# The low-part score products of the alone pairs on 64 rows of the array

## The chip, the cores and the metric

The kernel runs on one core of one Trainium2 chip. The metric is the device time of one execution in microseconds; the time of a kernel is the median of its runs.

## What is computed

Attention with capped scores over 4 x 12 heads, 448 positions and head width 64, followed by two gated products over all 1792 tokens. The reference, cut to what matters:

```python
scores = scale * np.matmul(q, k.transpose(0, 1, 3, 2))
scores = cap * np.tanh(scores / cap)
scores = scores - np.max(scores, axis=-1, keepdims=True)
attn = np.exp(scores)
attn = attn / (np.sum(attn, axis=-1, keepdims=True) + 1e-09)
x = np.matmul(attn, v)                      # heads put side by side: 1792 x 768

gate = 1.0 / (1.0 + np.exp(-(x @ w_gate)))  # 768 x 1536
x = (gate * (x @ w_val)) @ w_out            # 1536 x 768
h = x @ w_in                                # 768 x 2048
y = (h * np.cos(h)) @ w_out2                # 2048 x 768
```

All of it is float32.

## The kernel before

**Two parts for one number.** A float32 operand is split into a high part, rounded to the type fp32r, and a low part, the rest. A product of the gated stages is then three products on TensorE (`block3`: high x high, high x low, low x high).

**The scores** need only two, since the contraction is over 64 numbers and the array has 128 rows. `qk` brings q and k of a head twice, in partitions 0 to 63 and in 64 to 127. In place, q becomes (high part in partitions 0 to 63, low part in 64 to 127). This is done by one subtraction, L391: the tile `q_hi` is zero in partitions 0 to 63 and holds the high part of q in 64 to 127, and `q - q_hi` rounded to fp32r is just that. k becomes `k_hh` (the high part in both halves) and, in place, k's low part in both halves. A product with `k_hh` (L506) gives (q high + q low) x k high, a product with k's low part (L507) gives (q high + q low) x k low. Both contract over all 128 rows.

**Pairs, tiles, groups.** Two heads make a pair (`pr`, with d = 0, 1 for the head). The 896 queries of a pair are 7 tiles of 128; tile 3 (`MID`) takes the last 64 queries of either head, so it has products of both heads. The tiles go in groups (`GROUPS`): part 0 is tiles 0 and 1, part 1 tiles 2 and 3, part 2 tiles 4 and 5, part 3 tile 6. The scores of a group go into two PSUM banks, one for each tile (n = 0, 1), 448 columns each. Counted in products, a pair has 4 + 6 + 4 + 2 = 16.

**The alone pairs.** The six pairs of batch 0 (`pr < ALONE`) are worked on ahead of everything else, in steps of a software pipeline (`alone(m)`, one on each engine). In step m TensorE does the transposes of the first tile of group m-3, the scores of group m+1 (into `s_ps` or the first two banks of `acc`, in turn), products with v of an earlier pair (`times_v_alone`, plain float32, L561), and the transposes of the second tile. ScalarE takes tanh, then exp of every tile; VectorE takes the row maximum (L1091), the reciprocal of the sum, the normalisation (L1119) and a part of the copies of transposed tiles (L970), GpSimd the other normalisations and the splits of q and k. The later batches' pairs are worked on beside the gated products of the batch ahead; they call the same `scores`.

**Order and waits.** Each engine's order is as written, and semaphores tie the engines together. `scores` waits for the splits of the pair (`s_qk`, `s_first_low`), the caller for the tanh that frees the banks (`s_tanh`). GpSimd starts with the identity matrix for the transposes, then splits the second head of pair 0 and the first of pair 1. VectorE zeroes `q_hi` and splits the very first head. There is one `q_hi` for all pairs; GpSimd and VectorE alone use it. `z_hi` is a tile for the output of the second gated product, 128 partitions by 6 x 448 numbers, and is first written long after the alone pairs.

Of the kernel before, what the change touches and what calls it, by code (L numbers as in the profile page):

```python
# [11 lines left out]
ALU = mybir.AluOpType  # L12
# [3 lines left out]
B, H, S, D = 4, 12, 448, 64  # L16
DM = H * D
FF1, FF2 = 1536, 2048
P = 128
# [6 lines left out]
GROUPS = ((0, 1), (2, 3), (4, 5), (6,))  # L26
NG = len(GROUPS)
MID = 3
LAST = S // P * P
GAP = P - S % P  # L30

TURN = S - LAST
KW = TURN + S
# [7 lines left out]
ALONE = PAIRS  # L41
# [23 lines left out]
def build(nc, qk, v0, v, w1, w2, w3, w4, yT):  # L65

    def sb(name, shape, dtype=F32):
        return nc.alloc_sbuf_tensor(name, shape, dtype)
# [10 lines left out]
    def sem(name):  # L79
        return nc.alloc_semaphore(name)  # L80

    def f32(tile):
        return tile.bitcast(F32)
# [4 lines left out]
    z_hi, z_lo = sb("z_hi", [P, KD, S], F32R), sb("z_lo", [P, KD, S], F32R)  # L88
# [10 lines left out]
    k_hh = [[sb(f"k_hh{p}{d}", [P, KW], F32R) for d in range(2)] for p in range(2)]  # L99
    q_hi = sb("q_hi", [P, S + GAP], F32R)  # L100
# [8 lines left out]
    rowsum, guarded, recip = sb("rowsum", [P, TILES, 2]), sb("guarded", [P, TILES]), sb("recip", [P, TILES])  # L109

    prob_alone = [h_lo_whole[:, TILES * p:TILES * (p + 1), :] for p in range(2)]
    pt_alone = [h_hi_whole[:, 8 * p:8 * (p + 1), :].rearrange("p (c e) s -> p c (e s)", e=2) for p in range(2)]
# [17 lines left out]
    zeros = [bank[:, 511:512] for bank in o_ps]  # L132

    s_const, s_capd, s_zero, s_ident = sem("consts"), sem("cap_derived"), sem("ident_zeroed"), sem("ident_ready")
    s_pad = sem("zeros")
    s_wld = [[sem(f"w_whole_loaded{p}{h}") for h in range(2)] for p in range(LO)]
    s_whi, s_wsplit = sem("w_hi_done"), sem("w_split")
    s_hikept = [[sem(f"w_hi_kept{p}{h}") for h in range(2)] for p in range(HI)]
# [4 lines left out]
    s_khi, s_qhi, s_qk = [sem(f"k_hi_done{d}") for d in range(2)], [sem(f"q_hi_done{d}") for d in range(2)], [sem(f"qk_split{d}") for d in range(2)]  # L143
    s_first_kld, s_first_k = sem("k_of_first_head_loaded"), sem("k_hi_of_first_head")
    s_first_qhi, s_first_low = sem("q_hi_of_first_head"), sem("low_parts_of_first_heads")
    s_v0ld, s_vld = [sem(f"v_alone_loaded{d}") for d in range(2)], [sem(f"v_loaded{d}") for d in range(2)]
    s_vhi, s_v = [sem(f"v_hi_done{d}") for d in range(2)], [sem(f"v_split{d}") for d in range(2)]
    s_score, s_tanh, s_max, s_shift = sem("scores_done"), sem("tanh_done"), sem("max_done"), sem("shift_done")
# [17 lines left out]
    def keys(pr, d, of=qk_in):  # L166
        return of[pr % 2][d][:, K_AT[d]:K_AT[d] + KW]

    def queries(pr, d, of=qk_in):

        return of[pr % 2][d][:, KW:KW + S] if d == 0 else of[pr % 2][d][:, 0:S + GAP]

    def turned(pr, t):

        return t > MID if pr < ALONE else t in [ts[1] for ts in GROUPS if len(ts) > 1]

    def keys_of(pr, t):

        return slice(0, S) if turned(pr, t) else slice(TURN, KW)

    def tile_queries(pr, t, d):

        at = KW + P * t if d == 0 else LAST if t == MID else P * (t - MID - 1)
        return qk_in[pr % 2][d][:, at:at + P]

    def columns(pt, chunks, t):

        if t == MID:
            return pt[:, chunks, :].rearrange("p c (d s) -> p c d s", d=2)[:, :, :, LAST:S]
        at = P * t if t < MID else S + P * (t - MID - 1)  # L190
        return pt[:, chunks, at:at + P]
# [74 lines left out]
    with block:  # L266
# [114 lines left out]
        def _(e):  # L381
# [2 lines left out]
            e.affine_select(out=ident[:, :], in_=ident[:, :], compare_op=ALU.not_equal, fill=1.0,  # L384
                            base=0, pattern=[[-1, P]], channel_multiplier=1).then_inc(s_ident, 1)

            def rounded(out, in_):
                return e.tensor_scalar(out, in_, 1.0, 1.0, ALU.mult, ALU.mult)  # L388

            def rest(out, whole, hi):  # L390
                return e.tensor_tensor(out, whole, f32(hi), ALU.subtract)  # L391

            def qk_high(pr, d):

                q = queries(pr, d, qk_whole)
                e.wait_ge(s_qkld[pr % 2][d], 16 * (pr // 2 + 1))
                if pr == 0:
                    e.wait_ge(s_ident, 1)
                    e.wait_ge(s_first_low, 1)
                else:  # L400
                    rounded(k_hh[pr % 2][d][:, :], keys(pr, d, qk_whole)).then_inc(s_khi[d], 1)
                    e.wait_ge(s_khi[d], pr)
                rounded(q_hi[D:P, 0:q.shape[1]], q[D:P, :]).then_inc(s_qhi[d], 1)
                e.wait_ge(s_qhi[d], pr + d)

            def qk_low(pr, d):
                q = queries(pr, d, qk_whole)
                if pr > 0:
                    rest(keys(pr, d), keys(pr, d, qk_whole), k_hh[pr % 2][d][:, :])
                rest(queries(pr, d), q, q_hi[:, 0:q.shape[1]]).then_inc(s_qk[d], 1)  # L410

            def split_qk(pr, d):
                qk_high(pr, d)
                qk_low(pr, d)
# [9 lines left out]
            def split_v(pr, d):  # L424
                e.wait_ge(s_vld[d], 16 * (pr - ALONE + 1))
                if pr > ALONE:
                    e.wait_ge(s_pv, 2 * (pr - 1) + d + 1)
                rounded(v_hl[d][:, :, 0, :], v_raw[d][:, :, :]).then_inc(s_vhi[d], 1)
                e.wait_ge(s_vhi[d], pr - ALONE + 1)
                rest(v_hl[d][:, :, 1, :], v_raw[d][:, :, :], v_hl[d][:, :, 0, :]).then_inc(s_v[d], 1)  # L430
# [40 lines left out]
            for m in range(STEPS + 1):  # L471
                if m > 0:
                    normalise(m - 1)
                pr, d = divmod(m // 2 + 3, 2)
# [17 lines left out]
        def _(e):  # L492

            def scores(g, to):
                pr, part = divmod(g, NG)
                if part < 2:
                    if pr > 0 or part > 0:
                        e.wait_ge(s_qk[part], pr + part)
                    if pr == 0:
                        e.wait_ge(s_first_low, part + 1)  # L500
                for n, t in enumerate(GROUPS[part]):
                    heads = [d for d in range(2) if (t <= MID, t >= MID)[d]]
                    for d in heads:
                        q, last = tile_queries(pr, t, d), d == heads[-1]
                        k_hi, k_lo = k_hh[pr % 2][d], keys(pr, d)
                        e.matmul(to[:, n, 0:S], q, k_hi[:, keys_of(pr, t)], start=(d == heads[0]), stop=False)  # L506
                        m = e.matmul(to[:, n, 0:S], q, k_lo[:, keys_of(pr, t)], start=False, stop=last)  # L507
                m.then_inc(s_score, 1)

            def bank_is_free(x):  # L510
# [401 lines left out]
        @block.vector  # L912
        def _(e):
            e.memset(half_pi[:, :], math.pi / 2).then_inc(s_const, 1)
            e.memset(f32(q_hi)[0:D, :], 0.0).then_inc(s_pad, 1)
            for zero in zeros:
                e.memset(zero, 0.0).then_inc(s_pad, 1)
            e.memset(f32(qk_in[1][0])[:, KW + S:QK], 0.0).then_inc(s_pad, 1)
# [7 lines left out]
            first_keys(0)  # L926
            q = queries(0, 0, qk_whole)
            e.wait_ge(s_qkld[0][0], 16)
            e.tensor_scalar(q_hi[D:P, 0:S], q[D:P, :], 1.0, 1.0, ALU.mult, ALU.mult).then_inc(s_first_qhi, 1)
            e.wait_ge(s_first_qhi, 1)  # L930
            e.tensor_tensor(queries(0, 0), q, f32(q_hi)[:, 0:S], ALU.subtract).then_inc(s_first_low, 1)
            e.wait_ge(s_capd, 1)
            e.tensor_scalar(rowmax[:, :, 1], cap_abs[:, :].to_broadcast([P, TILES]), -1.0, None, ALU.mult).then_inc(s_const, 1)
            e.reciprocal(cap_inv[:, :], cap_abs[:, :]).then_inc(s_const, 1)
# [260 lines left out]
```

## Time and profile before

| | us |
|---|---|
| median of 3 runs | 1247.42 |
| lowest, highest | 1245.74, 1247.77 |
| the profiled execution | 1248.63 |
| its span, first to last instruction | 1246.8 |
| TensorE busy | 1233.1 |
| VectorE busy | 640.2 |
| ScalarE busy | 517.6 |
| GpSimd busy | 410.7 |
| end of the alone pairs | about 84 |

How to read the views: the page gives busy times over the whole span, the view by stretch the same for parts of it. The chain of waits follows the work that ended last back in time, and lists what it went through. The timeline lists single instructions. In it "PE" is a TensorE product and "PEld" the load of its weights, 128*128 the part of the array, and the shape behind it the output. A product's duration reaches from its start to the modelled end of its last column, so the products of a row overlap; the distance of two starts is what one costs. DVE is VectorE, ACT ScalarE, POOL GpSimd. The granted clock of TensorE is 1.00 in every stretch shown.

### The profile page before, as it was taken

How to read it: one execution, taken by the hardware profiler on the slowest of the kernel's cores; microseconds unless marked ns; L12 is line 12 of the kernel's file. 1: busy time of each engine (PE TensorE's matmuls, PEld its weight loads, DVE VectorE, ACT ScalarE, POOL GpSimd, SP SyncE). 2: the span in 40 equal slices, each digit the busy share in tenths (PEclk: the TensorE clock that was granted, in tenths of full speed). 3: DMA queues.
4: the chain of work that ended last, by engine and by line, in shares of the span. 5: the costliest groups of instructions: out<-in, count | busy, mean ns of one | idle time of the engine just before them, and what ended most of it. 6: DMA issues, size and time to landing. Idle time of an engine off the chain costs nothing.

```text
span 1246.8 us, 17228 instructions
## 1 busy us (share of the span) xinstructions
PE 1233.1 (99%) x6246; PEld 1120.9 (90%) x6246; DVE 640.2 (51%) x1332; ACT 517.6 (42%) x1051; POOL 410.7 (33%) x410
## 2 busy tenths in 40 slices
PE   7999999999999999999999999999999999999999
PEld 5779989999899999999999999999999999999998
DVE  6951158866772226876675212787666411114610
ACT  7941155555641116555652112665664111104510
POOL 7969968799653102322002300334100000000000
PEclk9999999999999999999999999999999999999999
DMA  4478986799677665456645665556654466666663
GB/s 153 159 239 317 321 299 233 257 329 327 231 277 277 212 222 193 168 204 233 249 159 197 234 224 205 176 192 229 223 218 173 143 233 213 218 215 216 243 234 113
DMA packets 100452, 279.19 MB, mean 224 GB/s; under 512 B 11152, under 2 KB 19600, under 8 KB 100368
## 3 DMA queue, kind: packets, MB, share of 16 engines
q1 hardware_dynamic: 96912, 272.58, 62.5%
q10 hardware_dynamic: 3456, 5.51, 1.2%
q8 instruction: 51, 0.84, 0.3%
q14 instruction: 33, 0.27, 0.1%
HBM read 219.05 MB, written 58.98 MB: 223 GB/s over the span
## 4 chain that ended last, share of the span: by engine, by line
PE 93%; DVE 3%; ACT 2%; issue 1%; DMA 0%; POOL 0%; SPq 0%; ACTq 0%
PE acc L592 26%; PE acc L591 26%; PE acc L593 26%; PE t_ps L543 3%; PE s_ps L506 2%; PE acc L581 2%; PE s_ps L507 2%; PE acc L561 2%; PE acc L583 2%; PE t_ps L527 1%; DMA qk_in_whole<-qk 0%; DVE rowmax L944 0%; ACT prob L752 0%; PE t_ps L545 0%; ACT h_lo_whole L773 0%
## 5 line engine op out<-in xcount | busy, mean ns | idle before, releaser
L591 PE MATMUL acc<-h_hi,w_hi 128*128 128x448 f32 x672 | 251.1, 374 | 0.0
L592 PE MATMUL acc<-h_lo,w_hi 128*128 128x448 f32 x672 | 245.8, 366 | 0.0
L593 PE MATMUL acc<-h_hi,w_lo 128*128 128x448 f32 x672 | 245.3, 365 | 0.0
L591 PE MATMUL acc<-x_hi,w_hi 128*128 128x448 f32 x576 | 211.3, 367 | 0.0
L593 PE MATMUL acc<-x_hi,w_lo 128*128 128x448 f32 x576 | 210.7, 366 | 0.0
L592 PE MATMUL acc<-x_lo,w_hi 128*128 128x448 f32 x576 | 210.7, 366 | 0.0
L1028 DVE SCALAR_TENSOR_TENSOR acc<-scratch,acc 128x448 f32<-128x448 f32 x48 | 30.2, 629 | 232.1 <-PE acc L593 232.0
L591 PE MATMUL acc<-z_hi,w_hi 128*128 128x448 f32 x384 | 140.7, 366 | 0.1
L593 PE MATMUL acc<-z_hi,w_lo 128*128 128x448 f32 x384 | 140.5, 366 | 0.0
L592 PE MATMUL acc<-z_lo,w_hi 128*128 128x448 f32 x384 | 140.5, 366 | 0.0
L593 PEld LDWEIGHTS acc<-h_hi,w_lo 128*128 128x128 f32 x672 | 126.3, 188 | 10.0
L591 PEld LDWEIGHTS acc<-h_hi,w_hi 128*128 128x128 f32 x672 | 126.4, 188 | 9.3
L592 PEld LDWEIGHTS acc<-h_lo,w_hi 128*128 128x128 f32 x672 | 126.5, 188 | 8.9
L391 POOL TENSOR_TENSOR w_lo<-w_lo_whole,w_hi 128x768 fp32r<-128x768 f32 (+1 forms) x64 | 125.1, 1954 | 5.3
L592 PEld LDWEIGHTS acc<-x_lo,w_hi 128*128 128x128 f32 x576 | 108.2, 188 | 9.2 <-issue 0.2
L593 PEld LDWEIGHTS acc<-x_hi,w_lo 128*128 128x128 f32 x576 | 108.2, 188 | 9.1
L591 PEld LDWEIGHTS acc<-x_hi,w_hi 128*128 128x128 f32 x576 | 108.2, 188 | 9.0 <-issue 0.2
L388 POOL TENSOR_SCALAR k_hh<-qk_in_whole 128x512 fp32r<-128x512 f32 x46 | 29.1, 633 | 241.0 <-DMA qk_in_whole<-qk 241.0
L830 ACT ACTIVATE h_hi<-acc 128x448 fp32r<-128x448 f32 x48 | 26.2, 545 | 178.6 <-DVE acc L1028 178.6
L758 ACT ACTIVATE prob<-prob,shift,cap_abs 128x448 f32<-128x448 f32 x126 | 94.6, 753 | 11.9 <-DVE shift L946 11.9
L944 DVE TENSOR_REDUCE rowmax<-prob 128x2 f32<-128x896 f32 x72 | 69.7, 968 | 55.7 <-ACT prob L752 55.6
L796 ACT ACTIVATE pt_hi<-t_ps 128x512 fp32r<-128x512 f32 (+1 forms) x126 | 68.3, 542 | 63.9 <-PE t_ps L543 38.4
(110 smaller groups left out, 2025.0 us busy)
## 6 DMA issues: line engine op xcount, KB each, us to landing
w_lo<-w_pair SPq DMA_DIRECT2D x156, 384.0 KB, 3.8
w_hi<-w_pair SPq DMA_DIRECT2D x156, 384.0 KB, 3.0
w_lo_whole<-w SPq DMA_DIRECT2D x52, 384.0 KB, 3.8
w_pair<-w_lo SPq DMA_DIRECT2D x52, 384.0 KB, 4.3
w_pair<-w_hi SPq DMA_DIRECT2D x52, 384.0 KB, 4.8
w_lo<-w_pair SPq DMA_DIRECT2D x36, 512.0 KB, 4.4
w_hi<-w_pair SPq DMA_DIRECT2D x36, 512.0 KB, 3.3
qk_in_whole<-qk SPq DMA_DIRECT2D x24, 512.0 KB, 5.7
```

Of the source, the lines that this page charges most:

```text
L388: return e.tensor_scalar(out, in_, 1.0, 1.0, ALU.mult, ALU.mult)
L391: return e.tensor_tensor(out, whole, f32(hi), ALU.subtract)
L506: e.matmul(to[:, n, 0:S], q, k_hi[:, keys_of(pr, t)], start=(d == heads[0]), stop=False)
L543: m = e.transpose(t_ps[x % 2][:, bass.ts(c, P)], p[:, first + c * P:first + (c + 1) * P], ident[:, :])
L591: e.matmul(out[:, 0:S], w_hi[u % HI][:, wb, :], a_hi[:, kb, :], start=first, stop=False)
L592: e.matmul(out[:, 0:S], w_hi[u % HI][:, wb, :], a_lo[:, kb, :], start=False, stop=False)
L593: return e.matmul(out[:, 0:S], w_lo[u % LO][:, wb, :], a_hi[:, kb, :], start=False, stop=last)
L758: e.activation(prob[:, t, :], prob[:, t, :], ACT.Exp, bias=shift[:, t:t + 1], scale=cap_abs[:, 0:1], accum_out=rowsum[:, t, 0:1]).then_inc ...
L796: e.activation(columns(pt_hi, slice(0, n), t), chunks_of(t_ps[x % 2], n, t), ACT.Copy).then_inc(s_pthi, 1)
L830: e.activation(h_hi[:, j, :], acc[2 + p][:, 0:S], ACT.Copy, scale=0.5).then_inc(s_hhi, 1)
L944: e.tensor_reduce(rowmax[:, at, 0], prob[:, at, :], AXIS_X, ALU.max).then_inc(s_max, 1)
L1028: e.scalar_tensor_tensor(acc[2 + p][:, 0:S], tmp_a[p], 1.0, acc[2 + p][:, 0:S], ALU.add, ALU.mult).then_inc(s_gated, 1)
```

## The change

In the alone pairs, in groups of two tiles, `scores` hands over to a new function `scores_alone`. It issues the products with the high part of k first, for all tiles of the group. Then it issues those with the low part, but over 64 rows only. Tile 0 of the group takes partitions 0 to 63: there q's high part lies in place. Tile 1 takes partitions 64 to 127, and there the high part of q comes from the rounded copy that `q_hi` held. (The product q low x k low falls away.) That copy must now last until TensorE has read it, so four areas of `z_hi` (`q_hi_alone`, two pairs by two heads) take the place of `q_hi` for the alone pairs. Their partitions 0 to 63 are zeroed once, in three of them and in `q_hi` by GpSimd, in one by VectorE, which formerly zeroed `q_hi`; two gaps of 64 columns in partitions 64 to 127 are zeroed too. The groups of one tile, and all pairs of later batches, stay as they were. The diff, without the signal's declaration:

```diff
+    q_hi_alone = [[z_hi.rearrange("p k s -> p (k s)")[:, (S + GAP) * (2 * p + d):(S + GAP) * (2 * p + d + 1)]
+                   for d in range(2)] for p in range(2)]
...
+    def tile_at(t, d):
+        return P * t if d == 0 else LAST if t == MID else P * (t - MID - 1)
+
     def tile_queries(pr, t, d):
-        at = KW + P * t if d == 0 else LAST if t == MID else P * (t - MID - 1)
+        at = tile_at(t, d) + (KW if d == 0 else 0)
         return qk_in[pr % 2][d][:, at:at + P]
+
+    def high_queries(pr, d):
+        return q_hi_alone[pr % 2][d] if pr < ALONE else q_hi
...
+            def zero(part):
+                return e.memset(f32(part), 0.0).then_inc(s_padp, 1)
+
+            zero(q_hi[0:D, :])
+            for n, (p, d) in enumerate(((0, 1), (1, 0), (1, 1))):
+                zero(q_hi_alone[p][d][0:D, :])
+            e.wait_ge(s_padp, 4)
+            for p in range(2):
+                zero(q_hi_alone[p][0][D:P, S:S + GAP])
+            e.wait_ge(s_padp, 6)
...
-                rounded(q_hi[D:P, 0:q.shape[1]], q[D:P, :]).then_inc(s_qhi[d], 1)
+                rounded(high_queries(pr, d)[D:P, 0:q.shape[1]], q[D:P, :]).then_inc(s_qhi[d], 1)
...
-                rest(queries(pr, d), q, q_hi[:, 0:q.shape[1]]).then_inc(s_qk[d], 1)
+                rest(queries(pr, d), q, high_queries(pr, d)[:, 0:q.shape[1]]).then_inc(s_qk[d], 1)
...
+                if pr < ALONE and len(GROUPS[part]) > 1:
+                    return scores_alone(g, to)
                 for n, t in enumerate(GROUPS[part]):
...
+            def scores_alone(g, to):
+                pr, part = divmod(g, NG)
+                work = [(n, t, d) for n, t in enumerate(GROUPS[part]) for d in range(2) if (t <= MID, t >= MID)[d]]
+                for n, t, d in work:
+                    e.matmul(to[:, n, 0:S], tile_queries(pr, t, d), k_hh[pr % 2][d][:, keys_of(pr, t)],
+                             start=(t != MID or d == 0), stop=False)
+                for n, t, d in work:
+                    rows = slice(0, D) if n == 0 else slice(D, P)
+                    q = tile_queries(pr, t, d) if n == 0 else high_queries(pr, d)[:, tile_at(t, d):tile_at(t, d) + P]
+                    m = e.matmul(to[:, n, 0:S], q[rows], keys(pr, d)[rows, keys_of(pr, t)],
+                                 start=False, stop=(t != MID or d == 1))
+                m.then_inc(s_score, 1)
...
-            e.memset(f32(q_hi)[0:D, :], 0.0).then_inc(s_pad, 1)
+            e.memset(f32(q_hi_alone[0][0])[0:D, :], 0.0).then_inc(s_pad, 1)
```

VectorE's split of the very first head writes to and subtracts `q_hi_alone[0][0]` in the same way.

TensorE, alone pair 2, parts 0 and 1, before (`qk_in00` holds q and, under the same name, k's low part of the first head, `k_hh00` its high part; `to` is `acc` and then `s_ps`):

```order
L506 MATMUL acc<-k_hh00,qk_in00 128x448
L507 MATMUL acc<-qk_in00 128x448
L506 MATMUL acc<-k_hh00,qk_in00 128x448
L507 MATMUL acc<-qk_in00 128x448
L561 MATMUL acc<-h_hi_whole_49,v_hl0_whole_58 128x448
L527 MATMUL t_ps0<-ident,h_lo_whole_50 128x128 x3
L527 MATMUL t_ps1<-ident,h_lo_whole_50 128x128 x3
L506 MATMUL s_ps<-k_hh00,qk_in00 128x448
L507 MATMUL s_ps<-qk_in00 128x448
```

The same place with the change (`z_hi` is the copy of q's high part):

```order
L541 MATMUL acc<-k_hh00,qk_in00 128x448 x2
L546 MATMUL acc<-qk_in00 128x448
L546 MATMUL acc<-qk_in00,z_hi 128x448
L601 MATMUL acc<-h_hi_whole_49,v_hl0_whole_58 128x448
L567 MATMUL t_ps0<-ident,h_lo_whole_50 128x128 x3
L567 MATMUL t_ps1<-ident,h_lo_whole_50 128x128 x3
L541 MATMUL s_ps<-k_hh00,qk_in00 128x448 x2
L541 MATMUL s_ps<-k_hh01,qk_in01 128x448
L546 MATMUL s_ps<-qk_in00 128x448
L546 MATMUL s_ps<-qk_in00,z_hi 128x448
L546 MATMUL s_ps<-qk_in01,z_hi 128x448
```

Within a group the low products have moved behind the high ones; the number of products and what stands around the group are the same.

GpSimd at the start of the kernel, before:

```order
L382 MEMSET ident 128x128
L384 ISA
L384 AFFINE_SELECT ident<-ident 128x128
L388 TENSOR_SCALAR q_hi<-qk_in01_whole_55 64x512
L391 TENSOR_TENSOR qk_in01<-qk_in01_whole_55,q_hi 128x512
```

And with the change:

```order
L394 MEMSET ident 128x128
L396 ISA
L396 AFFINE_SELECT ident<-ident 128x128
L400 MEMSET q_hi 64x512
L400 MEMSET z_hi 64x512 x3
L400 MEMSET z_hi 64x64 x2
L411 TENSOR_SCALAR z_hi<-qk_in01_whole_55 64x512
L414 TENSOR_TENSOR qk_in01<-qk_in01_whole_55,z_hi 128x512
```

Six memsets have come in ahead of the first split of q.

## Rows read from the trace of the kernel before

**Rows 1.** the page: busy time and share of each engine, then the clock by slice.
```profile
PE 1233.1 (99%) x6246; PEld 1120.9 (90%) x6246; DVE 640.2 (51%) x1332; ACT 517.6 (42%) x1051; POOL 410.7 (33%) x410
...
PEclk9999999999999999999999999999999999999999
```

**Rows 2.** busy time by stretch: us, busy and instructions of each engine, clock, DMA, GB/s.
```profile
25.60:69.60 44.00, 44.00 (x213) 31.86 (x214) 41.33 (x107) 40.46 (x86) 40.49 (x43) 1.00 0.51 165
69.60:76.80 7.20, 7.08 (x38) 4.51 (x37) 6.87 (x19) 5.54 (x14) 5.20 (x6) 1.00 0.65 204
76.80:84.10 7.30, 7.30 (x29) 4.08 (x27) 2.58 (x6) 1.14 (x2) 5.88 (x6) 1.00 0.72 258
84.10:1246.80 1162.70, 1157.43 (x5888) 1066.07 (x5886) 573.53 (x1157) 452.70 (x915) 341.28 (x332) 1.00 0.65 228
```

**Rows 3.** the chain of waits: start us, us, what; one group of part 0.
```profile
50.15 0.20 PE acc L506
50.35 0.20 PE acc L507
50.55 0.20 PE acc L506
50.76 0.20 PE acc L507
50.96 0.75 PE acc L561 x2
```

**Rows 4.** groups by line and form, TensorE, 25.6 to 69.6 us: busy us, mean ns | idle.
```profile
L506 PE MATMUL acc<-k_hh,qk_in 128*128 128x448 f32 x16 | 6.5, 407 | 0.0
L506 PE MATMUL s_ps<-k_hh,qk_in 128*128 128x448 f32 x15 | 6.1, 404 | 0.0
L507 PE MATMUL acc<-qk_in 128*128 128x448 f32 x16 | 5.8, 365 | 0.0
```

**Rows 5.** instructions in time, TensorE's weight loads: start us, us, line, operation.
```profile
49.88 0.19 PEld L506 LDWEIGHTS acc<-k_hh,qk_in 128*128 128x128 f32 x1
49.99 0.19 PEld L507 LDWEIGHTS acc<-qk_in 128*128 128x128 f32 x1
50.19 0.19 PEld L506 LDWEIGHTS acc<-k_hh,qk_in 128*128 128x128 f32 x1
```

**Rows 6.** instructions in time, TensorE's products, around a transpose on 128*64.
```profile
43.68 0.49 PE L527 MATMUL t_ps<-ident,h_lo_whole 128*128 128x128 f32 x3
44.01 0.27 PE L529 MATMUL t_ps<-ident,h_lo_whole 128*64 128x128 f32 x1
44.12 0.49 PE L527 MATMUL t_ps<-ident,h_lo_whole 128*128 128x128 f32 x3
```

**Rows 7.** waits, 25 to 70 us: who waited for whom, us in total, times, longest.
```profile
DVE h_hi_whole L970 <- PE t_ps L529: 1.3, 4, 0.3
...
ACT h_lo_whole L767 <- PE s_ps L507: 0.6, 3, 0.2
```

**Rows 8.** the chain of waits, 69 to 80 us.
```profile
70.01 0.69 DVE h_hi_whole L970
70.70 0.99 DVE rowmax L1091
...
75.83 0.55 PE t_ps L527 x3
```

**Rows 9.** instructions in time, all engines, the first groups.
```profile
7.64 0.63 ACT L744 ACTIVATE k_hh<-qk_in_whole 128x512 fp32r<-128x512 f32 x1 [3.41 <-DMA qk_in_whole<-qk]
...
8.18 0.99 ACT L767 ACTIVATE h_lo_whole<-acc,tanh_scale 128x896 f32<-128x896 f32 x1
...
10.22 0.44 PE L506 MATMUL s_ps<-k_hh,qk_in 128*128 128x448 f32 x1 [1.34 <-POOL qk_in L391]
...
11.72 1.01 ACT L767 ACTIVATE h_lo_whole<-s_ps,tanh_scale 128x896 f32<-128x896 f32 x1 [2.54 <-PE s_ps L507]
```

**Rows 10.** instructions in time, memsets and GpSimd's first split.
```profile
0.73 0.20 POOL L382 MEMSET ident<- 128x128 f32 x1 [0.29 <-POOLq L1189]
...
0.94 0.48 DVE L915 MEMSET q_hi<- 64x512 f32 x1
...
7.70 0.62 POOL L388 TENSOR_SCALAR q_hi<-qk_in_whole 64x512 fp32r<-64x512 f32 x1 [6.23 <-DMA qk_in_whole<-qk]
```

More of the change, by code:

```diff
@@ L134, in build @@
     s_const, s_capd, s_zero, s_ident = sem("consts"), sem("cap_derived"), sem("ident_zeroed"), sem("ident_ready")
-    s_pad = sem("zeros")
+    s_pad, s_padp = sem("zeros"), sem("zeros_by_pool")
     s_wld = [[sem(f"w_whole_loaded{p}{h}") for h in range(2)] for p in range(LO)]
@@ L928, in _ @@
             e.wait_ge(s_qkld[0][0], 16)
-            e.tensor_scalar(q_hi[D:P, 0:S], q[D:P, :], 1.0, 1.0, ALU.mult, ALU.mult).then_inc(s_first_qhi, 1)
+            e.tensor_scalar(q_hi_alone[0][0][D:P, 0:S], q[D:P, :], 1.0, 1.0, ALU.mult, ALU.mult).then_inc(s_first_qhi, 1)
             e.wait_ge(s_first_qhi, 1)
-            e.tensor_tensor(queries(0, 0), q, f32(q_hi)[:, 0:S], ALU.subtract).then_inc(s_first_low, 1)
+            e.tensor_tensor(queries(0, 0), q, f32(q_hi_alone[0][0])[:, 0:S], ALU.subtract).then_inc(s_first_low, 1)
             e.wait_ge(s_capd, 1)
```

## The prediction

> **What bounds the kernel now.** I read the page first. TensorE is busy for 99% of the span, VectorE for 51%, and the clock row shows nines throughout [rows 1]. Averages hide the stages, so the second view is the busy time by stretch [rows 2]. The alone pairs end at 84.1 us; the changed products all lie before that. They fall into four pieces. Up to 25.6 us TensorE has gaps. From 25.6 to 69.6 us it is busy for all 44.00 us, with VectorE at 41.33, ScalarE at 40.46 and GpSimd at 40.49. From 69.6 to 76.8 VectorE is the full one (6.87 of 7.20). From 76.8 to 84.1 TensorE is full again, but no scores are left there. The 1162.7 us behind it do not see the change and can only start earlier or later.
>
> Because busy time of TensorE has modelled ends, the third view is the chain of waits. Between 50.15 and 50.96 us it consists of nothing but the products of one group, one behind another [rows 3]: four products in 0.81 us, 0.203 us each. So in this stretch every 0.1 us taken from TensorE is 0.1 us off the chain, as long as VectorE, which has 44.00 - 41.33 = 2.7 us idle there, can follow.
>
> **How many products count.** Inside 25.6 to 69.6 us the groups by line show 16 + 15 high products of L506 and as many low ones of L507 [rows 4]. These are the 31 products of the groups 8 to 22. Three of them are one-tile groups, which the change leaves alone; 28 belong to 12 changed groups: 4 pairs, 3 groups each. A group of part 0 or 2 has two low products, one of part 1 three.
>
> **What the change does to one group.** Before: high, low, high, low, each a step of 0.203 us. After: the high ones first, then one low product on rows 0 to 63 and one (in part 1 two) on rows 64 to 127. No product is added or removed, and each still streams 448 columns. Whatever is gained is gained by two low products, in different halves of the array and different banks of PSUM, being in the array at once. Nothing in this trace shows two products at once, so I bound it. From above: the second costs nothing, 0.203 us less per group. From below: they follow each other as now, 0. The nearest rows for a value in between are those of the weight loads [rows 5]. A load starts when the product ahead of it starts (the loads at 49.99 and 50.19 us), and just behind the transposes, where the short product ahead does not hold it up, two loads follow each other after 0.11 us (49.88 to 49.99). The second low product needs weights of its own. If its load begins only when the first low product starts, it can start 0.11 us later, not 0.203. I take this: 0.203 - 0.11 = 0.093 us per group. Twelve groups give 1.1 us.
>
> **What it may cost: two changes of the array's split per group**, 128 rows to 64 and back, 24 in the 12 groups. The trace has no product on 64 rows. It has the nearest thing, a transpose on 128*64 of the array between others on 128*128 [rows 6]. They start at 43.68 (three of them), 44.01 and 44.12 us: 0.11 us a step into the narrow form and out of it, the same as between equals. By this row a change of form costs nothing, and that is the value I take. The other end: a product starts again only when the one ahead has left the array and its weights have been loaded with nothing above them. A product takes 0.365 us by its mean [rows 4] and 0.203 us in a row, so 0.16 us would come into view, with the load 0.27 us. A gain from a change of form is excluded, since a step cannot end before its columns have passed.
>
> The Trainium skill, page TensorEngine Tiling (Array Packing), section Key Properties, says that changing the tiling mode, not just the tile, drains TensorE. By that rule the sum turns over; it is the third rival. No row shows such a drain so far, and the narrow form of [rows 6] runs against it, but narrow in columns is not the same as split in rows.
>
> **Who follows.** With 1.1 us less on TensorE, VectorE would be idle for 1.6 us instead of 2.7 in that stretch. It still waits for transposes now, 1.3 us for L529 in four places [rows 7], so it is partly TensorE that holds it up, and I let the whole 1.1 us through. From 70.01 us the chain goes through VectorE (copy, row maximum, normalisation) until transposes at 75.83 [rows 8]. This block is as long as before and begins earlier by what TensorE gave.
>
> **The edits before 25.6 us.** Groups 0 to 7 run while other engines set the end. Group 1 alone stands on the chain: its six products from 10.22 us on end in the tanh at 11.72 us [rows 9]. It gives 0.1 us by the same reasoning, or costs up to 0.5 us with two changes of split. ScalarE takes group 0's tanh at 8.18 us, behind a copy of k that began at 7.64 when its load had landed, so that nothing follows from group 0 [rows 9]. The other groups have an idle TensorE behind them. GpSimd gets four memsets of 64x512 and two of 64x64 in front of its first split. The same shape took VectorE 0.48 us, and GpSimd needed 0.20 us for a 128x128 one [rows 10]. With 0.5 to 0.8 us each they take 2 to 3.5 us, and GpSimd now waits there for 6.23 us for a load. They are hidden at no cost; at over 1.5 us apiece they would not be, and each further one would be on the chain that leads to the product at 10.22 us. The two waits on their own counter stand on the same engine behind memsets already done, with only the split queued behind them. VectorE's memset is the old one with another target. The splits write the high parts of q to three further buffers and to the old one, same shapes, so GpSimd's and VectorE's work is the same, and TensorE's waits on it stand where they stood. No DMA is touched.
>
> **The sum.** 1.1 us in the full stretch, 0.1 us at group 1, nothing elsewhere: 1.2 us less. The profiled execution took 1248.63 us (its span 1246.8 and 1.8 around it) and would become 1247.4. It lies 1.2 us above the median of the three runs, 1247.42. Carried over to the median: 1246.2 us. What a measurement of this kernel can tell from no change is about 0.2%, 2.5 us: below 1244.9 is faster, above 1249.9 slower.
>
> **Rival 1: full overlap.** The weight load of the second low product is done in time, under the last high product, or both start together. For it: 0.203 us of cover and two loads of 0.11 us, which just about fits. Against it: every load in [rows 5] starts only with the product ahead of it. It gives 12 x 0.203 = 2.4 us, and about 1245.0, if VectorE's 2.7 us of idle time can really be used. The Trainium skill, page TensorE: Matmul & The Clock Gate, section Part 3: Packing small matmuls — row/col tiling, has products in distinct row groups start within 4 ns of each other, which is this rival; no row here shows such a pair.
>
> **Rival 2: nothing happens.** The two low products pass the array in turn and a change of split is free. The profile has no word against it, since only one product at a time is ever seen. 1247.4 us.
>
> **Rival 3, on the slower side: the change of split empties the array.** The place is each of the 24 boundaries in the full stretch. Price 0.16 to 0.27 us, so 3.9 to 6.5 us, plus 0.3 to 0.5 at group 1, less the 1.2 us of gain: +3.0 to +5.8, 1250.4 to 1253.2 us. From 0.05 us per boundary on the gain is gone (1.2 / 24), from 0.15 on the kernel is slower by more than 0.2%. For it: such a boundary has never occurred in this kernel, and the gain on the other side is small. Against it: the free narrow transposes of [rows 6].
>
> **How the numbers follow.** Forecast (late second load) 0.42; full overlap 0.20; nothing 0.13; emptied array 0.20; anything else, such as VectorE or a longer wait taking part of it or shortening more, 0.05. Predicted time 1246.2 us. Faster by over 0.2%: half of the full overlap, and a little of the forecast and the rest by scatter (the three runs lie 2 us apart), 0.15. Slower: the emptied array and a little more, 0.22. Within 0.2%: 0.63. The range takes in forecast, overlap and nothing, and the lower edge of the emptied array: 1244.7 to 1250.7 us.
>
> **What would show it.** In the changed profile, in the groups of pairs 2 to 5: the start of the low product on rows 64 to 127 relative to the one on rows 0 to 63 (0.11 us later by the forecast, nearly 0 by rival 1, 0.20 by rival 2). The step from the last high to the first low product, and from the last low one to the next instruction: 0.20 and below if the form is free, 0.36 or more if the array empties. The distance from the first product of a part 1 group to the L561 behind it: 6 x 0.203 = 1.22 us now, 1.13 by the forecast, 1.02 by rival 1, above 1.5 by rival 3. Moreover the end of the alone pairs: 84.1 now, 82.9 by the forecast. GpSimd's memsets should end before 5 us and its first split begin at about 7.7 us. It would be wrong altogether if TensorE showed new gaps behind VectorE or ScalarE in 25.6 to 69.6 us, or if a stage behind 84.1 us changed in length.

## The result and the profile after

The changed kernel takes 1248.76 us (median of 15 runs, 1247.71 to 1252.80), the kernel before 1246.35 us (15 runs, 1244.54 to 1247.77). The ratio is 1.0020, with a 95% interval of 1.0013 to 1.0027: slower, by about 2.4 us, where 1.2 us less had been forecast. The three runs that the prediction started from are among these fifteen; their median, 1247.42, lies 1.1 us above that of all.

The page of the changed kernel, busy times and the clock by slice (as [rows 1]), then its busy time by stretch, cut at the same events as [rows 2]: first product with v, last group of transposes held up by VectorE, resumption, first gated product.

```profile
PE 1234.8 (99%) x6246; PEld 1117.2 (90%) x6246; DVE 639.1 (51%) x1332; ACT 518.1 (42%) x1051; POOL 412.8 (33%) x416
...
PEclk8999999999999999999999999999999999999999
```

```profile
25.80:72.10 46.30, 46.29 (x212) 28.34 (x213) 41.52 (x107) 41.19 (x88) 40.37 (x43) 1.00 0.48 157
72.10:79.40 7.30, 7.17 (x38) 4.61 (x37) 6.78 (x19) 5.37 (x14) 5.12 (x6) 1.00 0.68 200
79.40:86.60 7.20, 7.20 (x28) 3.96 (x26) 2.50 (x6) 1.14 (x2) 5.80 (x6) 1.00 0.69 258
86.60:1246.50 1159.90, 1154.67 (x5888) 1066.21 (x5886) 572.39 (x1157) 452.97 (x915) 341.41 (x332) 1.00 0.65 228
```

The full stretch has grown from 44.0 to 46.3 us with the same work in it; the two behind it are as long as before within 0.1 us. The gated stages look 2.8 us shorter (1159.9 against 1162.7), which hides the loss in the two spans (1246.8 and 1246.5). The runs below show that this is no effect of the change. So from here on the yardstick is one span of time in each trace: from the first product with v to the first gated product, 84.06 - 25.59 = 58.47 us before, 86.58 - 25.81 = 60.77 us with the change.

The chain of waits of the changed kernel, a group of part 0 with the products with v behind it (as [rows 3]), then one of part 1:

```profile
51.50 0.41 PE acc L541 x2
51.92 0.40 PE acc L546 x2
52.32 0.95 PE acc L601 x2
53.27 0.65 PE t_ps L567 x6
53.92 0.61 PE s_ps L541 x3
54.54 0.61 PE s_ps L546 x3
```

Before, the four products and the two L561 took 0.81 + 0.75 = 1.56 us; now 0.41 + 0.40 + 0.95 = 1.76. The 0.20 us stands under L601, but it is not v's. The timeline of the same place, products and then weight loads (as [rows 5]), shows what it is:

```profile
51.26 0.66 PE L541 MATMUL acc<-k_hh,qk_in 128*128 128x448 f32 x2
51.85 0.46 PE L546 MATMUL acc<-qk_in 64*128 64x448 f32 x1
51.85 0.47 PE L546 MATMUL acc<-qk_in,z_hi 64*128 64x448 f32 x1
52.25 0.64 PE L601 MATMUL acc<-h_hi_whole,v_hl_whole 128*128 128x448 f32 x1
```

```profile
51.84 0.18 PEld L546 LDWEIGHTS acc<-qk_in 64*128 64x128 f32 x1 [0.31 <-issue]
51.85 0.18 PEld L546 LDWEIGHTS acc<-qk_in,z_hi 64*128 64x128 f32 x1
52.25 0.30 PEld L601 LDWEIGHTS acc<-h_hi_whole,v_hl_whole 128*128 128x128 f32 x2 [0.21 <-issue]
```

These rows show two things. The two low products start together, at 51.85 us, and so do their weight loads: full overlap. And no weight load is in flight ahead of either change of form: 0.31 and 0.21 us without one, where [rows 5] has the next load start with the product ahead. The first 64-row product lasts 0.46 us and not 0.365, the first 128-row one behind it 0.64 instead of 0.54. The load of weights, 0.11 us, has moved in front of them with nothing above it.

### The profile page after: what moved, and what is told of

The parts are those of the page before. It is cut to its first block, busy times and chain, and to the rows that moved or that the text cites. A ratio compares the mean times of both kernels' runs of the same rounds, so it can differ in the third digit from the quotient of the medians.

```text
span 1246.5 us, 17235 instructions
## 1 busy us (share of the span) xinstructions
PE 1234.8 (99%) x6246; PEld 1117.2 (90%) x6246; DVE 639.1 (51%) x1332; ACT 518.1 (42%) x1051; POOL 412.8 (33%) x416
## 4 chain that ended last, share of the span: by engine, by line
PE 93%; DVE 3%; ACT 2%; issue 1%; DMA 0%; POOL 0%; SPq 0%; ACTq 0%; POOLq 0%
PE acc L631 26%; PE acc L632 26%; PE acc L633 26%; PE t_ps L583 3%; PE acc L601 2%; PE acc L621 2%; PE s_ps L531 2%; PE s_ps L532 2%; PE acc L623 2%; PE t_ps L567 1%; DMA qk_in_whole<-qk 0%; DVE rowmax L984 0%; ACT prob L792 0%; PE t_ps L585 0%; ACT h_lo_whole L813 0%
## 5 line engine op out<-in xcount | busy, mean ns | idle before, releaser
L798 ACT ACTIVATE prob<-prob,shift,cap_abs 128x448 f32<-128x448 f32 x126 | 94.6, 753 | 11.9 <-DVE shift L986 11.9
L984 DVE TENSOR_REDUCE rowmax<-prob 128x2 f32<-128x896 f32 x72 | 69.7, 968 | 56.3 <-ACT prob L792 56.3
```

The source lines that it names most:

```text
L798: e.activation(prob[:, t, :], prob[:, t, :], ACT.Exp, bias=shift[:, t:t + 1], scale=cap_abs[:, 0:1], accum_out=rowsum[:, t, 0:1]).then_inc ...
L984: e.tensor_reduce(rowmax[:, at, 0], prob[:, at, :], AXIS_X, ALU.max).then_inc(s_max, 1)
```

## The experiments

All times of the yardstick come from the timelines. From the third row on, the ratio is to runs of the kernel before on the same chip at the same time, whose medians were 1246.1 to 1246.7 us. The first product with v and the first gated product are read from one profile of each kernel.

| kernel | first product with v | first gated product | between | median, us | ratio to before |
|---|---|---|---|---|---|
| before | 25.59 | 84.06 | 58.47 | 1246.35 | |
| the change | 25.81 | 86.58 | 60.77 | 1248.76 | 1.0020 (1.0013 to 1.0027) |
| before again | 25.40 | 83.87 | 58.47 | 1246.74 | 1.0002 (0.9993 to 1.0010) |
| buffers only | 25.57 | 84.04 | 58.47 | 1246.39 | 1.0002 (0.9993 to 1.0011) |
| order only | 24.22 | 82.74 | 58.52 | 1247.10 | 1.0005 (0.9997 to 1.0014) |
| one half | 27.99 | 92.62 | 64.63 | 1253.36 | 1.0054 (1.0038 to 1.0069) |
| low first | 25.63 | 86.51 | 60.88 | 1248.38 | 1.0015 (1.0005 to 1.0024) |
| low x3, 64 rows | 25.95 | 93.17 | 67.22 | 1255.87 | 1.0074 (1.0060 to 1.0087) |
| low x3, 128 rows | 27.15 | 96.95 | 69.80 | 1259.19 | 1.0101 (1.0087 to 1.0115) |
| products in the gap | 25.58 | 86.42 | 60.84 | 1248.76 | 1.0018 (1.0009 to 1.0027) |
| interleaved | 31.95 | 102.67 | 70.72 | 1262.38 | 1.0130 (1.0114 to 1.0145) |
| the change again | 25.54 | 86.34 | 60.80 | 1248.14 | 1.0017 (1.0008 to 1.0027) |

### Before again

No edit.

> The kernel before once more, for its own scatter and for a second trace. Theory A (the price of the change lies in the alone pairs alone: 2 changes of the array's split per group at 0.20 us each, one product of 0.203 us saved, 12 groups, 2.4 us): the first gated product starts at about 84.1 us again, and what differs behind it between the two traces on hand (the gated stages of the kernel before took 2.8 us longer than those of the changed one in the profiled executions) is scatter and will differ here too. Rival B (the buffers in z_hi or the shifted start make the gated stages faster): products of the gated stages take 206.7 ns a step from 100 to 170 us here again, as in the first trace of before, and 202.7 with the change. Median within 0.1% of before.

58.47 us again. Its gated stages took 1160.0 us (span 1243.9), as long as those of the changed kernel, so the 2.8 us are scatter of the kernel before itself. The other way round, the kernel with products in the gap, which has the whole change, took 1163.1 us there, and the second profile of the change 1159.8. Rival B is out. Where the 2.8 us are is seen when the same stretch of time is read in the profile first shown of the kernel before, in that of the changed kernel and in this run (us, busy and count of each engine). TensorE is full in all three, with 341, 347 and 347 products:

```profile
100.00:170.00 70.00, 70.00 (x341) 63.72 (x340) 15.29 (x27) 13.21 (x25) 62.14 (x54) 1.00 0.90 312
```

```profile
100.00:170.00 70.00, 70.00 (x347) 64.88 (x346) 14.91 (x26) 13.11 (x24) 62.48 (x54) 1.00 0.92 322
```

```profile
100.00:170.00 70.00, 70.00 (x347) 64.86 (x347) 15.81 (x27) 14.53 (x28) 62.91 (x53) 1.00 0.92 318
```

### Buffers only

The changed kernel without its products:

```diff
-                if pr < ALONE and len(GROUPS[part]) > 1:
-                    return scores_alone(g, to)
```

> The change without its products: q's high parts in the four new areas, the six memsets, but all score products in the old order and on 128 rows. Theory A: no difference, first gated product at 84.1 us, clock 1.00 throughout, median within 0.1% of before. Rival C (the memsets on GpSimd or the other buffers cost): first gated product later than 84.6 us.

58.47 us, first gated product at 84.04; rival C is out. One part of the forecast missed: the granted clock was at 0.50 for 3.4 us from 15.8 us on, as in the second profile of the kernel before. GpSimd's memsets (in the changed kernel) end near 3.6 us, well before its first split. This part of the prediction holds, with a larger margin than assumed: the timeline of GpSimd in the changed kernel gives 0.52 us for the first and 1.74 for the other five together.

```profile
1.41 0.52 POOL L400 MEMSET q_hi<- 64x512 f32 x1
1.86 1.74 POOL L400 MEMSET z_hi<- 64x512 f32 x5
7.76 0.61 POOL L411 TENSOR_SCALAR z_hi<-qk_in_whole 64x512 fp32r<-64x512 f32 x1 [4.15 <-DMA qk_in_whole<-qk]
```

### Order only

The changed kernel with its low products on all rows:

```diff
-                    rows = slice(0, D) if n == 0 else slice(D, P)
-                    q = tile_queries(pr, t, d) if n == 0 else high_queries(pr, d)[:, tile_at(t, d):tile_at(t, d) + P]
+                    rows = slice(0, P)
+                    q = tile_queries(pr, t, d)
```

> The change's order (high products of a group first, then the low ones), but the low products on all 128 rows. Theory A: no change of split, nothing saved: 0.203 us a product, first gated product at 84.1 us, like before. Rival D (the order itself, four weight loads of another sequence, costs the 0.2 us per group): 86.5 us. On the clock: if it falls to half at 16 us here too, the order is what lets it fall; if it stays at 1.00, the overlap and the emptied array are (the same columns are streamed here as before).

58.52 us: rival D is out. The order costs nothing. The whole start came 1.3 us earlier in this profile, because the load that GpSimd's first split waits for landed earlier; the timeline has the split at 6.40 us, not at 7.76:

```profile
6.40 0.62 POOL L411 TENSOR_SCALAR z_hi<-qk_in_whole 64x512 fp32r<-64x512 f32 x1 [2.78 <-DMA qk_in_whole<-qk]
```

The medians do not show a gain from it, so this too is scatter, of the loads. The granted clock stayed at 1.00 from 5.3 us on. By the expectation the overlap and the changes of form would then be what lets it fall in the changed kernel; other runs contradict this, since it fell in two profiles that have neither (before again, buffers only) and stayed at 1.00 in one that has both (low x3, 64 rows).

### One half

The changed kernel with all its low products in rows 0 to 63:

```diff
-                    rows = slice(0, D) if n == 0 else slice(D, P)
-                    q = tile_queries(pr, t, d) if n == 0 else high_queries(pr, d)[:, tile_at(t, d):tile_at(t, d) + P]
+                    rows = slice(0, D)
+                    q = tile_queries(pr, t, d)
```

> The low products on 64 rows, but all of them in the same half, rows 0 to 63. Theory A: the changes of split stay (0.40 us per group), the overlap goes: 12 x 0.40 = 4.8 us over before in the stretch where TensorE is the bound, first gated product at 84.1 + 4.8 + about 0.2 = 89.1 us, 2.4 us more than with the change; the low products start 0.2 us apart. Rival E (the 64-row form is slow in itself, the overlap saves nothing): no later than with the change, 86.6 us.

64.63 us, 3.9 more than with the change and 6.2 more than before, where 4.8 had been expected. The chain, a group of part 0 and the high and low products of one of part 1:

```profile
56.12 0.41 PE acc L541 x2
56.53 0.60 PE acc L546 x2
57.13 0.95 PE acc L601 x2
58.08 0.65 PE t_ps L567 x6
58.73 0.60 PE s_ps L541 x3
59.34 0.80 PE s_ps L546 x3
```

The group with its v products takes 0.41 + 0.60 + 0.95 = 1.96 us: 0.40 over before, 0.20 over the change. That is the expected price and, for the overlap, the expected gain. The low products start 0.31 us apart at first, since the first of them still waits for its weights, and 0.20 us apart from then on. The rest, 1.4 us, is the granted clock: it was at half (0.50 in the view by stretch) from 17.0 to 30.7 us in this run, so that the first 2.7 us of the measured span ran at the lower level, and 2.7 us at half speed lose 1.35. The first gated product, expected at 89.1 us, came at 92.62, because the first product with v was late too (27.99 us). Rival E is out. Its view by stretch, with the clock third from the end:

```profile
17.00:30.00 13.00, 12.46 (x38) 8.67 (x38) 11.14 (x29) 11.07 (x24) 12.35 (x15) 0.50 0.20 57
31.00:40.00 9.00, 9.00 (x40) 5.45 (x39) 5.89 (x18) 7.05 (x14) 4.72 (x7) 1.00 0.26 82
```

### Low first

The changed kernel with the two loops of `scores_alone` exchanged (flags of the first and last product with them):

```diff
+                for n, t, d in work:
+                    rows = ...
+                    e.matmul(to[:, n, 0:S], q[rows], keys(pr, d)[rows, keys_of(pr, t)],
+                             start=(t != MID or d == 0), stop=False)
                 for n, t, d in work:
-                    e.matmul(to[:, n, 0:S], tile_queries(pr, t, d), k_hh[pr % 2][d][:, keys_of(pr, t)],
-                             start=(t != MID or d == 0), stop=False)
-                for n, t, d in work:
...
+                    m = e.matmul(to[:, n, 0:S], tile_queries(pr, t, d), k_hh[pr % 2][d][:, keys_of(pr, t)],
+                             start=False, stop=(t != MID or d == 1))
```

> As the change, but the low products of a group come ahead of its high ones. Theory A (each change of split costs a drain and a weight load that nothing hides): on the way in, the instruction ahead is now a transpose of 128 columns, whose step (0.11 us) is set by its weight load and not by its columns, so less of the wait is new: about 0.16 us instead of 0.20; on the way out 0.20 as before, now in front of the high products. So +0.16 us a group instead of +0.20, 12 groups 1.9 us over before instead of 2.3 in the stretch from the first product with v to the first gated product (60.4 us; before 58.5, with the change 60.8). Rival F (leaving or entering 64 rows costs a fixed time whatever stands ahead): 60.8.

60.88 us: theory A's 60.4 missed, rival F's number. What stands ahead of a change of form, a transpose of 128 columns or a product of 448, makes no difference that shows. The theory had held that a transpose leaves less to wait for. The rows of before say otherwise: a transpose lasts 0.27 us at a step of 0.11 ([rows 6]), a high product 0.365 at 0.203, so either goes on for 0.16 us beyond its step. In this run the first low product starts 0.20 us behind the last transpose, 0.09 more than the step of 0.11. The chain of this run puts the extra 0.20 us elsewhere and leaves the sum: group and v products 0.41 + 0.60 + 0.75 = 1.76 us.

```profile
51.35 0.41 PE acc L543 x2
51.76 0.60 PE acc L546 x2
52.37 0.75 PE acc L601 x2
```

### Low products three times, on 64 and on 128 rows

The low products of a group are gone through three times in turn, not each three times in a row: tile 0, tile 1, tile 0, tile 1 and so on, so that the halves alternate. The second kernel has the same edit on top of the order-only one:

```diff
-                for n, t, d in work:
+                for i, (n, t, d) in enumerate(work * 3):
                     rows = ...
...
-                                 start=False, stop=(t != MID or d == 1))
+                                 start=False, stop=(i >= 2 * len(work) and (t != MID or d == 1)))
```

> The change with every low product of its groups issued three times in a row (the low part is added three times, so the scores are not the reference's). Theory A: between two changes of split the halves overlap fully, so that a pair of low products costs 0.203 us: 12 groups have 16 such slots, 2 x 16 x 0.203 = 6.5 us more than with the change in the stretch from the first product with v to the first gated product: 67.3 us, and 2.6 us less than the same on 128 rows. Rival G (overlap only for the first pair behind a change of split): 2 x 28 x 0.203 = 11.4 us more, 72 us.

> The same repetition of every low product, but on all 128 rows, in the change's order (the low part is added three times here too). Both theories: 2 x 28 x 0.203 = 11.4 us more than the order alone in that stretch, 69.9 us. Theory A puts it 2.6 us above the 64-row form, rival G 2 us below.

67.22 and 69.80 us, both within 0.1 of theory A; rival G is out. With three pairs between two changes of form (in a group of part 1, nine low products in six slots) the 64-row shape wins by 2.6 us, with one pair it loses 2.3. The timeline of the 64-row kernel shows the pairs, 0.30 us behind the high product and then at 0.20 us a pair:

```profile
48.88 0.36 PE L541 MATMUL acc<-k_hh,qk_in 128*128 128x448 f32 x1
49.17 0.47 PE L546 MATMUL acc<-qk_in 64*128 64x448 f32 x1
49.18 0.47 PE L546 MATMUL acc<-qk_in,z_hi 64*128 64x448 f32 x1
49.48 0.36 PE L546 MATMUL acc<-qk_in 64*128 64x448 f32 x1
49.49 0.36 PE L546 MATMUL acc<-qk_in,z_hi 64*128 64x448 f32 x1
49.68 0.36 PE L546 MATMUL acc<-qk_in 64*128 64x448 f32 x1
49.69 0.36 PE L546 MATMUL acc<-qk_in,z_hi 64*128 64x448 f32 x1
```

### Products in the gap

The changed kernel with 12 small products where TensorE idles near 14 us:

```diff
             for m in range(STEPS + NG + 2):
                 alone(m)
+                if m == 2:
+                    busy(12)
```

> The change with 12 products of 128 columns on the identity matrix put in where TensorE idles from about 13.4 to 15.3 us, ahead of the first transposes; their results are overwritten. Theory A: the granted clock stays at 1.00 where it fell to 0.50 from 16 to 23 us with the change, and that gives back only what the half clock put on the chain there, about 0.2 us; the 2.3 us of the full stretch stay, first gated product near 86.3 us. Rival H (the half clock is the main price of the change): near 84.3 us.

60.84 us. The granted clock was at half earlier here, from 11.9 to 15.3 us, and at full from then on, where the changed kernel had it at 0.50 from 16 to 23 us. It fell before the products that were put in began (13.85 us), so the run does not say what lets the clock fall. The inserted products (24 records for the 12) also filled more than the gap: the first transposes started at 17.21 us instead of 15.35. The view by stretch:

```profile
12.00:15.00 3.00, 3.00 (x11) 2.26 (x11) 1.90 (x5) 3.00 (x7) 2.92 (x4) 0.50 0.51 164
...
16.00:23.00 7.00, 6.45 (x44) 4.58 (x42) 5.72 (x18) 7.00 (x16) 6.83 (x9) 1.00 0.30 102
```

It does say that rival H is out: with the full clock from 15.3 us on the first product with v came at 25.58 instead of 25.81 us, and the 2.3 us of the full stretch were all there. The timed runs agree: ten of the eleven have a mean clock of 0.999 or 1.000, and their median, 1248.76 us, is still 2.1 above that of the kernel before.

### Interleaved

64 rows and alternate halves, but in the order of before:

```diff
-                for n, t, d in work:
-                    e.matmul(to[:, n, 0:S], tile_queries(pr, t, d), k_hh[pr % 2][d][:, keys_of(pr, t)],
-                             start=(t != MID or d == 0), stop=False)
                 for n, t, d in work:
                     rows = slice(0, D) if n == 0 else slice(D, P)
                     q = ...
+                    e.matmul(to[:, n, 0:S], tile_queries(pr, t, d), k_hh[pr % 2][d][:, keys_of(pr, t)],
+                             start=(t != MID or d == 0), stop=False)
                     m = e.matmul(to[:, n, 0:S], q[rows], keys(pr, d)[rows, keys_of(pr, t)],
```

> The low products on 64 rows in alternate halves as with the change, but in the old order: high, low, high, low. Theory A (every change of split costs 0.20 us by itself, and a low product on 64 rows else as much as on 128): 4 changes in a group of part 0 or 2, 6 in one of part 1, so 14 x 0.20 = 2.8 us per pair and 11.2 us in the 4 pairs of the full stretch, with no overlap; stretch from the first product with v to the first gated product 58.5 + 11.2 = 69.7 us. Rival I (what costs is going back to 128 rows behind a pair of overlapped products, not the change of split as such): 0.2 us per group as with the change, at most 63 us.

70.72 us. Rival I is out. As in the one-half run the clock was still at half for the first 2.8 us of the measured span, 1.4 us, so that 69.3 remain against 69.7 expected. In the chain every step from the first low product on takes 0.40 us, whichever way the form changes; the way out of the last one stands under L600 (1.70 us for four, 1.50 without it):

```profile
52.32 0.21 PE s_ps L543
52.52 0.39 PE s_ps L545
52.92 0.40 PE s_ps L543
53.32 0.40 PE s_ps L545
53.71 0.40 PE s_ps L543
54.11 0.40 PE s_ps L545
54.51 1.70 PE acc L600 x4
```

### The change again

> The change once more, for a second trace: theory A expects 60.8 us from the first product with v to the first gated product again; the first product with v and the gated stages may lie otherwise by 1 to 3 us, as in the traces of the kernel before.

60.80 us. The granted clock was at 0.50 for 6.8 us again, from 14.4 us on.

## Why the prediction was wrong

Its reading of the kernel holds. The full stretch is bound by TensorE, what is added there comes out at the end of the alone pairs (12 groups, +2.3 us between the two marks, +2.5 at the first gated product), VectorE's block behind it keeps its length, the memsets and buffers cost nothing, and the order costs nothing. Two terms of the sum were wrong.

**The step that failed is the price of a change of form**, taken as nothing from [rows 6]. Measured, it is 0.20 us each way, 0.40 us a group. This alone turned a gain into a loss. The working, from the rows above: behind the last high product (48.88) the first low one starts 0.29 to 0.30 us later instead of 0.20, and then lasts 0.47 instead of 0.36 us, because its weights are loaded only then; 0.10 + 0.10. That this is a price per change and not per group is what the interleaved kernel shows (4 or 6 changes a group) and the one-half kernel (2 changes, nothing saved: 0.40). It lies inside the prediction's other end, 0.16 to 0.27 us, though its parts are other ones: of the 0.16 us for an emptying array 0.10 came into view, of the load, 0.11, about all. So the sign set for an emptied array, a step of 0.36 us or more from the last high to the first low product, did not appear (0.29 to 0.30), nor did the other, 0.20; the rest of the price stands in the longer first product. For the same reason the distance from a part 1 group to its L601 (1.39 us by the starts; 1.30 before, where the prediction had 1.22 from the steps) met none of the values given for it: half of the price of the way out lies in the product behind.

The choice rested on a transpose on 128*64. That is narrow in columns and has all the rows, and by its steps it is not a change of form in this sense. In the changed kernel's timeline it still costs nothing, a few hundred nanoseconds from 64-row products that do:

```profile
44.85 0.49 PE L567 MATMUL t_ps<-ident,h_lo_whole 128*128 128x128 f32 x3
45.18 0.27 PE L569 MATMUL t_ps<-ident,h_lo_whole 128*64 128x128 f32 x1
45.29 0.49 PE L567 MATMUL t_ps<-ident,h_lo_whole 128*128 128x128 f32 x3
```

The Trainium skill, page TensorEngine Tiling (Array Packing), section Key Properties, which the prediction cited as speaking against the change, has a change of the tiling mode drain TensorE. For rows this case's traces agree that the change costs: 0.20 us, half of it a later start, half the load. The Trainium skill, page TensorEngine Tiling (Array Packing), section Available Configurations, counts 128x64 among the modes. If the 128*64 of the profile is that mode, the trace shows no such cost for a change in columns.

**The overlap was sized too small**, 0.093 us a group instead of 0.203. The second weight load was assumed to wait for the first low product; the two loads and the two products start within 0.01 us of each other. (A small misreading besides: the load at 49.99 us in [rows 5] starts 0.08 us behind the product ahead of it, which the timeline has at 49.91, and not with it. Nothing in the sum hangs on this.) This is rival 1 and what the Trainium skill, page TensorE: Matmul & The Clock Gate, section Part 3: Packing small matmuls — row/col tiling, says of distinct row groups.

So neither the forecast nor one rival came true. What happened is rival 1's full overlap together with rival 3's price per boundary, which the prediction had priced apart: per group 2 x 0.20 - 0.203 = +0.20 us, times 12 = 2.4 us, against 2.3 measured between the marks and 2.4 in the medians. Rival 3 had set only the small gain against the drain, and so landed higher, at +3.0 to +5.8. The direction was wrong. The measured time lies inside the stated range, but that is luck: the range reached up to 1250.7 us to take in the lower edge of rival 3, and no line of the prediction gives +2.4 us. By its own marks the result is at the border between no change and slower: 1248.76 us is below 1249.9, and the ratio to the kernel before is 1.0020.

**At the start** the sixfold group 1 was to give 0.1 us or cost 0.5. It did neither: its six products and the tanh behind them stand at 10.20 and 11.69 us (10.22 and 11.72 in [rows 9]). A product of 0.203 us was saved and one change of form, the way in, paid; the way out falls behind the product that tanh waits for. The first product with v came 0.2 us later in one trace of the change and on time in the other. The granted clock was at 0.50 for 6.8 us there, in a part where TensorE has slack, which the prediction did not foresee:

```profile
14.00:16.00 2.00, 0.66 (x5) 0.58 (x5) 1.75 (x5) 2.00 (x6) 1.83 (x3) 1.00 0.76 247
17.00:22.00 5.00, 4.54 (x16) 2.97 (x17) 4.15 (x12) 4.60 (x11) 4.83 (x7) 0.50 0.00 0
23.00:25.00 2.00, 2.00 (x15) 1.48 (x14) 1.77 (x7) 1.89 (x6) 1.92 (x3) 1.00 0.46 181
```

TensorE had been idle for 1.93 us before 15.35 us, as it had been before (1.92 us) without a fall. The kernel before, run again, had a fall of 3.4 us near 16 us and reached its first product with v no later (25.40 us). The timed runs show that the longer fall goes with the change: all 25 of the changed kernel have a mean clock of 0.996 or 0.997, where the 63 of the kernel before beside the experiments spread from 0.997 (14 of them) to 1.000 (23). The former average 1246.8 us and the latter 1246.3, 0.5 us apart, with runs of either group scattered by about 1 us. Between the marks, where the 2.3 us are, the clock is 1.00 in both kernels. What lets it fall is open. It mattered only in the one-half and the interleaved kernels, where it reached into the full stretch.

No version that beats both kernels came out of this. By the same sum two pairs of low products between two changes of form break even (2 x 0.203 saved against 0.40), which was not run, and three gain, as the run of three shows, and a group has one pair, with other full-array work on both sides. Two groups together would have five low products in three slots, two saved, again even; this was worked out and not run.

## What to carry to other kernels

Splitting the array by rows pays per pair of overlapped products and costs per change of form. Here one 448-column product was saved for each pair and 0.20 us paid for each change, so by the sum fewer than three pairs between two full-array instructions gain nothing. This is measured for fp32r products of 448 columns; other widths were not run. When the trace lacks an operation, the nearest row decides only if it is like the missing one in the respect that matters: a product narrow in columns said nothing on one split in rows, and the bound worked out from a product's duration and its weight load held the measured price.

## What the runs showed of the hardware that was not expected

- Two 64-row products on different halves and banks start within 0.01 us of each other, weight loads included, and a pair passes at the step of one (0.20 us); three pairs in a row keep that.
- A change between 128 and 64 rows costs 0.20 us either way (steps of 0.40 us in the interleaved kernel), whether a transpose of 128 columns (low first) or a product of 448 (the change) stands ahead. Between products on 64 rows the half can change at no cost (0.20 us a pair in low x3, as in a row of full-array products).
- Streaks of full-array products run at one of two steps, 0.207 or 0.203 us, in the same granted clock of 1.00. From 100 to 170 us the first profile of before has 341 of them, the changed kernel and before again 347: 6 x 0.203 = 1.2 us in 70. Four of the twelve profiles have the slow step there (before, buffers only with 342, low x3 on 64 rows, products in the gap), with the change and without it. Which one a stretch gets was not settled. The gated stages took 1159.7 to 1163.1 us over the twelve profiles, and the first loads landed up to 1.4 us apart; either can hide what the change moved.
